# Three small moves at the start of an attention and two-block kernel: an order of transfers, an order of table columns, one warm-up product

## The reference, cut to what matters

```python
def _attn_ref(q, k, v, n_global, n_local):            # q, k, v: 2 x 8 heads x 768 x 64
    scores = scale * np.matmul(q, k.transpose(0, 1, 3, 2))
    rel = pos[:, None] - pos[None, :]
    is_global = pos[None, :] < int(n_global)          # 8
    is_local = (rel >= 0) & (rel < int(n_local))      # 96
    keep = is_global | is_local
    dist = np.where(is_global & ~is_local, float(n_local), np.abs(rel))
    scores = np.where(keep, scores - slopes[:, None, None] * dist, -1e9)
    a = softmax(scores)
    return np.matmul(a, v)
# x = attention output as 1536 x 512
# block 1: h = x @ w_in (512 x 1024); solu = h * softmax(h); layer norm * g_ln; @ w_out
# block 2: h = x @ w_in (512 x 2048); (h * sigmoid(h)) @ w_out
```

## Time and profile before

| | |
|---|---|
| three runs, us | 488.73, 488.76, 489.19 |
| profiled execution, its own time, us | 488.78 |
| its span, us | 486.8 |
| PE busy, us | 479.8 |
| DVE busy, us | 302.1 |
| ACT busy, us | 273.2 |
| POOL busy, us | 220.3 |
| granted clock of TensorE, mean | 1.0 |

### The profile page before, as it was taken

How to read it: one execution, slowest core, us unless ns; L and a number is a source line. 1 busy time by engine, 2 the same in 40 slices (tenths; PEclk the granted TensorE clock), 3 DMA queues, 4 the chain that set the end, 5 groups by cost and what they waited for, 6 DMA issues and landing times.

```text
span 486.8 us, 8013 instructions
## 1 busy us (share of the span) xinstructions
PE 479.8 (99%) x2758; PEld 413.3 (85%) x2758; DVE 302.1 (62%) x729; ACT 273.2 (56%) x607; POOL 220.3 (45%) x288
## 2 busy tenths in 40 slices
PE   8999999999999999999999999999999999999997
PEld 5667888888888888889889888989999988988995
DVE  6987756576566676665475657655475446545542
ACT  5988556576566566845754455454463454344422
POOL 6435409669668779232614441344225431344200
PEclk9999999999999999999999999999999999999999
DMA  8992012641551551202222201222026201220003
GB/s 232 299 268 71 2 49 55 160 126 40 158 135 46 144 143 41 107 0 88 95 80 88 87 25 63 86 88 82 5 85 220 87 15 72 88 86 2 0 1 129
DMA packets 20202, 44.38 MB, mean 91 GB/s; under 512 B 2560, under 2 KB 8128, under 8 KB 20160
## 3 DMA queue, kind: packets, MB, share of 16 engines
q1 hardware_dynamic: 20000, 43.47, 29.3%
q10 hardware_dynamic: 160, 0.37, 0.3%
HBM read 40.69 MB, written 3.15 MB: 90 GB/s over the span
## 4 chain that ended last, share of the span: by engine, by line
PE 96%; ACT 2%; DMA 1%; DVE 1%; issue 0%; SPq 0%; ACTq 0%; DVEq 0%
PE hidden_ps L1186 24%; PE x_ps L1021 14%; PE hidden_ps L972 11%; PE score_ps L1209 9%; PE x_t_ps L959 5%; PE x_t_ps L1209 5%; PE x_ps L1209 5%; PE probs_t_ps L1209 5%; PE turn_ps L1209 5%; PE probs_t_ps L923 4%; PE hidden_ps L989 2%; PE turn_ps L1002 2%; PE score_ps L912 2%; PE score_ps L894 1%; PE score_ps L893 1%; ACT probs L1289 1%
## 5 line engine op out<-in xcount | busy, mean ns | idle before, releaser
L869 POOL TENSOR_TENSOR wo_lo<-w_raw,wo_hi 128x512 fp32r<-128x512 f32 x32 | 41.4, 1316 | 145.5 <-ACT wo_hi L1456 145.5
L1468 ACT ACTIVATE act_hi<-mix_c 128x384 fp32r<-128x384 f32 x64 | 33.7, 526 | 96.5 <-DVE mix_c L1847 96.1
L727 POOL TENSOR_SCALAR probs<-probs,exp_inv 128x232 f32<-128x232 f32 x72 | 34.6, 497 | 50.5 <-DVE exp_inv L1618 48.7
L1289 ACT ACTIVATE probs<-logits,low_logit 128x232 f32<-128x232 f32 x96 | 45.5, 477 | 3.0 <-DVE low_logit L1605 2.7
L1847 DVE TENSOR_TENSOR mix_u<-hidden_ps,mix_p 128x384 f32<-128x384 f32 x16 | 8.9, 558 | 57.0 <-PE hidden_ps L1186 57.0
L1021 PE MATMUL x_ps<-w_out_hi,u_hi 128*128 128x512 f32 x96 | 40.6, 423 | 0.0
L1852 DVE TENSOR_TENSOR act_lo<-mix_c,act_hi 128x384 fp32r<-128x384 f32 x64 | 36.1, 566 | 6.3 <-ACT mix_c L1469 5.5
L1021 PE MATMUL x_ps<-w_out_hi,u_lo 128*128 128x512 f32 x96 | 37.8, 394 | 0.0
L1021 PE MATMUL x_ps<-w_out_lo,u_hi 128*128 128x512 f32 x96 | 37.6, 391 | 0.0
L972 PE MATMUL hidden_ps<-w_in_hi,x_hi 128*128 128x512 f32 x80 | 33.0, 412 | 0.0
L1605 DVE CUSTOM_DVE_ANT_0 logits<-score_ps,bias 128x232 f32<-128x232 f32 x88 | 30.6, 395 | 3.5 <-issue 3.5
(11 more groups left out here) (215 smaller groups left out, 1445.0 us busy)
## 6 DMA issues: line engine op xcount, KB each, us to landing
w_raw<-w SPq DMA_DIRECT2D x16, 1024.0 KB, 4.9
v_sb<-v_win SPq DMA_DIRECT2D x22, 224.0 KB
late_k_raw<-k_t SPq DMA_DIRECT2D x16, 232.0 KB, 4.3
k_raw<-k_t SPq DMA_DIRECT2D x14, 232.0 KB, 3.7
out<-out_sb SPq DMA_DIRECT2D x12, 256.0 KB, 2.1
w_in_raw<-w_in SPq DMA_DIRECT2D x4, 512.0 KB, 7.6
w_out_raw<-w_out SPq DMA_DIRECT2D x4, 512.0 KB, 11.2
late_q_raw<-q_t SPq DMA_DIRECT2D x16, 128.0 KB, 4.0
```

The costliest lines, as they stand in the source:

```text
L727: last = nc.gpsimd.tensor_scalar(probs[p][:, e, :], probs[p][:, e, :], exp_inv[:, p, e:e + 1], 0.0, ALU.mult, ALU.add)
L869: nc.gpsimd.tensor_tensor(wo_lo[j % 2][:, c, :], w2_raw[j % 2][:, c, BANK:2 * BANK], wo_hi[j % 2][:, c, :].bitcast(F32), ALU.subtract).the ...
L1289: last = nc.scalar.activation(probs[p][:, e, :], logits[b][:, e, :], ACT.Exp, scale=-1.0, bias=low_logit[:, b, e:e + 1], accum_out=exp_sum ...
L1468: nc.scalar.activation(act_hi[c][:, :], mix_c[c][:, :], ACT.Silu)
```

## The change

SP issues tile 0's key piece first, then the spans, then the query piece. ACT writes all four pairs' table columns before the first exponents. `keep_warm(8)` becomes `keep_warm(7)`.

```diff
-    def load_first(eng, unit):
+    def load_first(eng, unit, between=None):
         rows = slice(unit * DH, unit * DH + DH)
         eng.dma_start(staged_k_raw[rows, :], k_v[0, unit]).then_inc(early_loaded[0], 16)
+        if between is not None:
+            eng.dma_start(spans_i[:, :], between).then_inc(spans_loaded, 16)
         eng.dma_start(staged_q_raw[rows, :], q_v[0, unit]).then_inc(early_loaded[0], 16)
...
-            sp.dma_start(spans_i[:, :], spans).then_inc(spans_loaded, 16)
-            load_first(sp, 1)
+            load_first(sp, 1, spans)
             load_early(1)
...
             pe.wait_ge(zeros_made, 1)
-            keep_warm(8)
+            keep_warm(7)
             early_scores(0, 0)
...
             def first_steps():
-                first_table(2)
-                first_table(3)
                 exps(0, 1)
...
             load_first(act, 0)
             first_table(0)
             first_table(1)
+            first_table(2)
+            first_table(3)
             exps(0, 0)
```

## The result

The changed kernel takes 490.33 us (median of nine runs, 490.14 to 490.47), the kernel before 489.04 us beside it (nine runs, 488.53 to 490.01). The ratio is 1.0026, with a 95% interval of 1.0018 to 1.0035: slower by 0.26%, some 1.3 us, where +0.6 was forecast. The profiled executions, 490.43 and 488.78, lie 1.65 us apart. The three first runs of before (median 488.76) were from the low end of what that kernel does; more runs gave medians of 488.95 to 489.33.

What follows compares the result with a forecast made beforehand. PE, busy 479.8 of 486.8 us, was taken as the bound, with the change acting only ahead of 17.51. Spans' delay 2.0 less 1.42 gave 0.58, the product 0: 488.78 + 0.58 = 489.36 us, range 488.4 to 490.1.

Steps and rivals of the forecast that it cites:

- The path of a delay: A delay or gain reaching ACT's exponents of tile 0 passes to PE at 17.51, then nearly one for one to the end.
- Part 1: Spans issued behind SP's key piece: landing at 4.3, 2.0 us later, bounded by 2.9 and 4.85; first table at 7.57.
- the delay less 1.42: At the third pair's exponents, the change costs the spans' delay minus 1.42 us, not under -0.24: 0.58 us later.
- Rival (b): Spans' delay passes 2.4 us, as their completion also waits for ACT's query piece: 489.8 to 490.3; chance 0.13.
- the cover named: Queries landing up to 0.3 earlier or later don't count: scores done at 7.2, first mask waits until 8.1, 0.9 us cover.
- POOL, set at nothing: POOL's table work ends at 10.9, some 0.3 us late, but only a late DVE copy uses its transposes: counted nothing.
- Part 2: Tables 2 and 3 ahead of the first exponents: 0.80 us moved, free if spans are on time.
- the cap: Tables' gain limited to 0.24 us, as `exps(0, 2)` waits for `mask(0, 2)` behind a reciprocal that does not move.
- Part 3: One zero product less before tile 0's scores: PE ends 0.44 us sooner, worth nothing; clock rises between 5.2 and 7.8.
- Rival (c): Clock falls as PE waits about 1.6 us for its first transposes: +1.0 to +1.5 on top, about 490.6; chance 0.08.

Runs made afterwards that it cites:

- nine products: Nine zero products in place of eight, else the kernel before: 489.31 us against 489.25, ratio 0.9999.
- seven products: One zero product less alone, keep_warm(7) for keep_warm(8), on the kernel before: 489.54 us, ratio 1.0004.
- tables alone: Tables of pairs 2 and 3 ahead of the first exponents, spans first, eight zero products, against the kernel before: 489.31 us, ratio 1.0001.
- spans at 1.3, own queue empty: SP issues spans first but only near 1.3, ACT's keys at 0.73, tables ahead, eight zero products, against the kernel before: 489.68 us, ratio 1.0009.
- order, tables (8 products): The changed kernel with its eighth zero product back: 490.57 us, ratio 1.0026 to the kernel before.
- order alone: Only the order of SP's transfers changed on the kernel before, tables and eight zero products kept: 490.65 us against 489.33, ratio 1.0026.
- the kernel whose scores were held back on purpose: SP's order as in the changed kernel, eight zero products, ACT holds its two pieces back until the spans land: 493.58 us in one run.
- POOL's split one place later: Two kernels, POOL's second weight split behind late_table(2), with and without the tables' move, against before: 489.33 us (1.0006) and 489.66 us (1.0009).
- two places later: POOL's second weight split behind both late tables, with the tables' move, against the kernel before: 489.05 us beside 489.03, ratio 0.9998.

## Why the prediction was wrong, step by step

**The path of a delay: right.** Twelve profiles give one line. The last column is the profiled time less the start of tile 0's last value product:

| kernel | spans at DVE | first mask | last value product | time | less |
|---|---|---|---|---|---|
| before | 2.52 | 7.30 | 17.51 | 488.78 | 471.27 |
| before again | 2.52 | 7.24 | 17.37 | 488.80 | 471.43 |
| before again | 2.52 | 7.43 | 17.57 | 488.85 | 471.28 |
| nine products | 2.55 | 7.92 | 18.06 | 489.31 | 471.25 |
| seven products | 2.56 | 8.28 | 18.41 | 489.58 | 471.17 |
| tables alone | 2.60 | 7.35 | 17.66 | 488.80 | 471.14 |
| spans at 1.3, own queue empty | 4.46 | 8.17 | 18.60 | 489.79 | 471.19 |
| order, tables (8 products) | 5.25 | 8.95 | 18.95 | 490.34 | 471.39 |
| changed kernel | 5.32 | 9.02 | 19.03 | 490.43 | 471.40 |
| order alone | 5.42 | 9.12 | 19.26 | 490.61 | 471.35 |
| order, tables (8 products) | 5.55 | 9.25 | 19.25 | 490.61 | 471.36 |
| changed kernel again | 5.63 | 9.34 | 19.33 | 490.72 | 471.39 |

Whatever moved the last value product, the time followed within 0.3 us, so no slack shows between it and the end (the other five profiles have 471.28 to 471.50). From first mask to that product it is 10.1 us with the second tables between the exponents, 9.9 to 10.0 with them in front, plus what DVE's small instruction waits for POOL.

**Part 1, the spans behind the key piece: the step that failed.** I took a landing at 4.3 and let it reach 4.85 at most; it was 5.29 in the profile and up to 5.6 in another. The form was right (the cost is the delay less 1.42), the term was too small: delay 2.8 in place of 2.0, which makes 1.38 in place of 0.58, and 0.1 more as the first mask follows the table's start by 0.64 and not 0.55 us: 1.5, as measured at the exponent. (The 0.64 was never read before, as PE released that mask then.) The landing missed the forecast by 0.99 us, at 5.29 for 4.3. The bound was wrongly made. I took the spans to land soon after the key piece of their own queue, and wrote "ACT's 232 KB beside" without charging for them, although in the rows of before the piece that went second took the longer 3.8. Two pieces were ahead, not one. And I added 0.3 us for the packets' movement but let the landing follow at the quiet pace: they took 0.64, and the completion 1.06. Rival (b), at a chance of 0.13, came nearest: it had the other queue's traffic in it, and its price, 489.8 to 490.3, ends where the measured median lies. But the piece that it named isn't the one. It had the completion wait for ACT's query piece, whose last packet was over at 5.40, after the spans had landed; what stood ahead was ACT's key piece.

The landing of the queries was not earlier but 0.3 later, at 6.33, inside the cover named.

**POOL, set at nothing: 0.1 us.** The working had POOL late by some 0.3 us and used only by a DVE copy that was late too. The copy waits 0.15 us for it, and what follows comes 0.1 later for that.

**Part 2, the tables: right in the cap, wrong in its reach.** 0.17 of the 0.24 came at the exponent, and in the profile DVE's wait for POOL took it. With the spans late the tables ahead save 0.1 from mask to product, which is hardly to be told in the medians (490.57 against 490.65).

**Part 3, the product: nothing, as forecast.** But "so the clock rises between 5.2 and 7.8" was taken from one profile as if it were a property. It rose ahead of the scores (6.0 to 6.5) in some executions, at about 7, 10 or 11 us in others; seven products had it early once and late twice, eight had it both ways, nine at 7. Rival (c) expected a fall after the wait at 11 us; the three zero products there took 0.94 us, as before, so the clock was high by then. No row read shows it fall; it was late.

**The measured size.** The mechanism costs 1.5 us against a favourable run of before and less against one whose first scores wait for the clock or the queries; that is why the medians have 1.3.

## What to carry to other kernels

Price a small transfer by everything issued ahead of it on every queue, plus the slower packets and completion under load, and move it behind bulk only if its own consumer chain has that much slack: here 1.4 us of slack, 2.8 of delay. Find the first instruction that all later work follows (the table above) and measure experiments there, to 0.1 us, where medians of runs can't tell 0.4. And when a profile looks calm at a spot that depends on the clock's rise, take a second one before a margin is built on it.

## What the runs showed of the hardware

- Landing of 2 KB: 1.6 to 1.8 us with nothing ahead, 3.0 to 3.1 behind one 232 KB piece on either queue, 3.9 to 4.2 behind two. The first packets of the pieces of both queues start one behind the other in order of issue: in the changed kernel SP's keys at 2.08, ACT's keys at 2.87, the spans at 3.59.
- TensorE's rise from the 1.2 to the 2.4 GHz level (zero products 0.44 and 0.23 us apart) came anywhere from about 5 us (spans at 1.3: the last two zero products took 0.65 us, 1.05 in the kernel with the order alone) to about 11 us, with PE working from 0.99 us on and no gap over 1.7 us ahead of the scores (the kernel whose scores were held back on purpose aside). The granted clock reads 1.00 in the windows of before and after that were read; only the spacing shows it.
- A DVE tensor_scalar of four elements a row took 0.17 us where POOL's running instruction was over within 0.15 us of its start, and lasted until 0.02 us after the end of POOL's where that came later, in six profiles (before 0.32, tables alone 0.57, spans at 1.3 0.57, POOL's split one place later 0.81 and 0.81, two places later 0.27). The Trainium skill, "SBUF — State Buffer", "SBUF: two separate sides", says that DVE, in a mode with two ports, and GpSimd share a port pair which whoever starts first holds for its whole instruction, while the other blocks; these rows agree. That this small instruction runs in such a mode no row shows.
